# Decayed attention in a fused attention and two-MLP kernel: units of 64 steps of four batches on 64x64 tiles, and loops written out

## The reference

```python
def _attn_ref(r, k, v, w, u):            # (4, 8, 768, 48): batch, heads, steps, width
    for t in range(S):
        cur = einsum('bhd,bhe->bhde', u[None] * kt, vt)
        y[:, :, t] = einsum('bhd,bhde->bhe', rt, state + cur)
        state = wt[:, :, :, None] * state + einsum('bhd,bhe->bhde', kt, vt)
```

## Time and profile before

| | us |
|---|---|
| median of 3 runs | 892.63 (889.56 to 893.0) |
| span of the profiled execution | 889.9 |
| TensorE busy | 804.8 (90%), granted clock 0.973 |
| DVE, ACT, POOL busy | 527.3, 427.7, 181.4 |
| ACT's copies into `r_diag` | 116.6 (168 of them) |

### The profile page before, as it was taken

The page is one execution under the profiler, slowest core; times in us unless marked ns, Lnnn a source line. Parts: engine busy times, 40 slices in busy tenths (PEclk is TensorE's granted clock), DMA queues, the critical chain, the costliest instruction groups (busy, mean ns, idle before and its releaser), DMA issues.

```text
span 889.9 us, 23575 instructions
## 1 busy us (share of the span) xinstructions
PE 804.8 (90%) x9648; PEld 667.1 (75%) x9648; DVE 527.3 (59%) x906; ACT 427.7 (48%) x716; POOL 181.4 (20%) x189
## 2 busy tenths in 40 slices
PE   2365958999999999999999999899999999999998
PEld 2254848779779779779778778678878778887786
DVE  5657384783883883683783683584584674453333
ACT  4536354673573573473473473363463573342332
POOL 5223222221221221221221221132132131000000
PEclk9978887999999999999999999899999999999999
DMA  5140345147535434334434434344434432333653
GB/s 179 36 124 3 91 162 120 49 145 180 189 127 170 165 123 127 128 126 127 152 112 130 140 111 125 109 144 136 131 108 133 138 140 90 123 127 107 235 190 106
DMA packets 33971, 114.75 MB, mean 129 GB/s; under 512 B 5840, under 2 KB 14544, under 8 KB 33872
## 3 DMA queue, kind: packets, MB, share of 16 engines
q1 hardware_dynamic: 33872, 113.27, 40.7%
HBM read 91.23 MB, written 17.30 MB: 122 GB/s over the span
## 4 chain that ended last, share of the span: by engine, by line
PE 73%; DVE 12%; issue 6%; ACT 4%; POOL 1%; SPq 1%; DMA 1%; DVEq 0%; ACTq 0%; POOLq 0%
PE hid L492 20%; PE acc L505 17%; PE flex L476 12%; PE flex L445 10%; PE flex L375 3%; PE flex L413 3%; PE flex L416 3%; PE flex L459 2%; DVE r_t L618 2%; DVE att L600 2%; DVE solu L659 2%; PE flex L427 1%; ACT att L815 1%; DVE ln_lo L687 1%; DVE w_up L627 1%
## 5 line engine op out<-in xcount | busy, mean ns | idle before, releaser
L492 PE MATMUL hid<-y_hi,w 128*128 128x512 f32 x576 | 198.8, 399 | 3.2 <-DVE y_lo L694 3.2
L505 PE MATMUL acc<-g_hi,w 128*128 128x512 f32 x576 | 197.2, 396 | 1.4 <-DVE g_lo L703 0.9
L815 ACT ACTIVATE r_diag<-r_t 64x512 f32<-64x512 f32 (+1 forms) x168 | 116.6, 694 | 105.8 <-DVE r_t L618 89.7
L699 DVE TENSOR_TENSOR act<-act 128x512 f32<-128x512 f32 x96 | 73.6, 766 | 125.3 <-ACT g_hi L815 125.3
L1010 POOL TENSOR_TENSOR k_t<-k_t,w_up 128x512 f32<-128x512 f32 x72 | 87.4, 1213 | 220.5 <-PE flex L375 160.6
L492 PEld LDWEIGHTS hid<-y_hi,w 128*128 128x128 f32 x576 | 109.0, 189 | 27.2 <-issue 3.6
L505 PEld LDWEIGHTS acc<-g_hi,w 128*128 128x128 f32 x576 | 108.1, 188 | 26.6 <-issue 2.8
L815 ACT ACTIVATE act<-hid 128x512 f32<-128x512 f32 x96 | 57.3, 597 | 135.1 <-PE hid L492 134.9
L492 PE MATMUL hid<-y_lo,w 128*128 128x512 f32 x288 | 113.3, 393 | 0.0
L505 PE MATMUL acc<-g_lo,w 128*128 128x512 f32 x288 | 112.6, 391 | 0.0
L476 PE MATMUL flex<-ln_hi,out_hi 128*128 128x256 f32 x288 | 82.8, 288 | 0.0
(11 more groups left out here) (98 smaller groups left out, 1348.5 us busy)
## 6 DMA issues: line engine op xcount, KB each, us to landing
w<-split_w SPq DMA_DIRECT2D x80, 768.0 KB, 4.4
split_w<-w SPq DMA_DIRECT2D x16, 768.0 KB, 4.1
r_t<-in_rT SPq DMA_DIRECT2D x24, 192.0 KB, 4.9
k_t<-in_kT SPq DMA_DIRECT2D x24, 192.0 KB, 4.7
w_t<-in_wT SPq DMA_DIRECT2D x24, 192.0 KB, 5.6
v_n<-in_vN SPq DMA_DIRECT2D x12, 384.0 KB, 3.3
out<-o_stage SPq DMA_DIRECT2D x5, 768.0 KB, 4.1
x_pack<-x_t SPq DMA_DIRECT2D x72, 48.0 KB, 2.4
```

The source lines that it names most:

```text
L492: last = mm(hid[:, :], w2[:, j % RING, w, k * P:(k + 1) * P], y[:, k, :], start=n == 0, stop=n == len(terms) - 1)
L505: last = mm(acc[:, d], w2[:, j % RING, w, rows], gx[:, j % 2], start=j == 0 and n == 0, stop=j == J2 - 1 and n == 2, skip_group_check=True)
L699: e.tensor_tensor(act[:, j % 2], act[:, j % 2], act[:, j % 2], ALU.mult).then_inc(g_ready, 1)
L815: return nc.scalar.activation(out_, in_, func, **more)
```

## The change

A unit becomes 64 steps of all four batches: `T` = 64, `NU` = 12 units, `Q` = 16 blocks of 64 columns, six levels. All tiles keep their number of columns, the state loses its axis of pairs, and each unit now decays and updates all of it. `r_diag`, `att_bk`, `right_halves`, `take_level5`, `take_level6` and `place_blocks` go. The matmuls of the bonus and the levels read `r_t` and `k_t` themselves, one head each, on tiles of 64 rows and 64 columns; the head chooses the PSUM bank, the parity of `q` the column half. DVE masks each level (512 elements a partition, before 256; the bonus 1024, before 512) straight into `att`. `carry(l)` now stands behind `pair_scores(l)` and waits for the matmuls of its own level. One of the two output copies goes to ACT; `k_natural` waits for the last level's scores, `output` for both halves of k, `state_step` for both output copies. The first MLP's and the second MLP's matmuls stay as they are. The loops over blocks 1 to 3 are written out on every engine.

```diff
-T = 128
-LEVELS = 7
+T = 64
+LEVELS = 6
-LEVEL_AT = {1: 0, 3: 1, 4: 2, 6: 3, 7: 4, 8: 5, 9: 6}
+LEVEL_AT = {1: 0, 3: 1, 4: 2, 6: 3, 7: 4, 8: 5}
+        def scores(q, i):
+            return flex[HALF * (q % 2):HALF * (q % 2 + 1), i, q // 2 * T:(q // 2 + 1) * T]
...
             def bonus(u):
                 pe.wait_ge(uk_ready, u + 1)
-                pe.wait_ge(rdiag_ready, u * 14 + 2)
-                wait(pe, x_ready, u * 2)
+                pe.wait_ge(r_in, (u + 1) * 32)
+                wait(pe, state_ready, u * 2)
                 for q in range(Q):
...
+                    steps = slice(q * T, (q + 1) * T)
                     for i in range(2):
                         rows = slice(HALF * i, HALF * (i + 1))
+                        last = mm(scores(q, i), uk[rows, steps], r_t[rows, steps], start=True, stop=True)
+                last.then_inc(bonus_mm, 1)
+            def level(u, l):
+                if l == 0:
+                    pe.wait_ge(bonus_taken, u + 1)
+                else:
+                    pe.wait_ge(r_ready, u * LEVELS + l)
+                    pe.wait_ge(k_ready, u * LEVELS + l)
+                    pe.wait_ge(level_taken, u * LEVELS + l)
+                for q in range(Q):
+                    steps = slice(q * T, (q + 1) * T)
+                    for i in range(2):
+                        rows = slice(HALF * i, HALF * (i + 1))
+                        out_ = scores(q, i)[:, 0:T // 2].rearrange("p (n m) -> p n m", m=1 << l)
+                        last = mm(out_, k_t[rows, steps], halves(r_t[rows, steps], l)[:, :, 1, :], start=True, stop=True)
+                last.then_inc(level_mm, 1)
...
+            def output(u):
+                pe.wait_ge(r_ready, u * LEVELS + LEVELS)
+                pe.wait_ge(vn_in, (u + 1) * 16)
+                pe.wait_ge(knat_ready, (u + 1) * 2)
+                for q in range(Q):
+                    x, b2 = q // 2, q % 2
+                    for i in range(2):
+                        mm(flex[HALF * i:HALF * (i + 1), b2, x * T:(x + 1) * T], state[:, q, i], r_t[:, q * T:(q + 1) * T],
+                           start=x == 0, stop=False, skip_group_check=True)
+                for q in range(Q):
+                    x, b2 = q // 2, q % 2
+                    rows = slice(HALF * b2, HALF * (b2 + 1))
+                    for i in range(2):
+                        last = mm(flex[HALF * i:HALF * i + D, b2, x * T:(x + 1) * T], v_n[rows, x % NBH, head_cols(x, i)],
+                                  att[rows, i, x], start=False, stop=x == NX - 1, skip_group_check=True)
...
             def pair_scores(u, l):
...
+                v.wait_ge(level_mm, u * LEVELS + l + 1)
+                keep = mask[:, off:off + pairs].bitcast(U32).unsqueeze(1).unsqueeze(3).broadcast_to([P, Q, pairs, 1 << l])
                 e.copy_predicated(dst, keep, src).then_inc(level_taken, 1)
...
             def carry(u, l):
...
-                v.wait_ge(rdiag_ready, u * 14 + 2 * l + 2)
...
+                v.wait_ge(level_mm, u * LEVELS + l + 1)
                 right = halves(r_t[:, :], l)[:, :, 1, :]
...
             def attention(u, g, i):
-                if i in CARRY_AT:
-                    carry(u, CARRY_AT[i])
...
+                if i == 0:
+                    bonus_scores(u)
+                elif i in LEVEL_AT:
+                    pair_scores(u, LEVEL_AT[i])
+                    carry(u, LEVEL_AT[i])
...
-            with pe.Fori(1, NC - 2) as m:
+            for m in range(1, NC - 2):
                 block_turns(m)
```

More of the change, by code:

```diff
@@ L92, in build @@
         out_hi, out_lo = sb("out_hi", [P, J1, DM], F32R), sb("out_lo", [P, J1, DM], F32R)
-        state = sb("state", [P, G, Q, 2, HALF])
+        state = sb("state", [P, Q, 2, HALF])
         u_rows = sb("u_rows", [P, NP])
@@ L221, in load_r @@
             def load_r(u):
-                wait(sp, y_mm, u * 2)
+                wait(sp, y_mm, u)
                 for i in range(2):
@@ L365, in level @@
-                bank = flex[:, l % 2]
-                for q in range(Q):
[L367 to L384, removed]
@@ L398, in k_natural @@
                     last.then_inc(knat_mm, 1)
-            def output(u, g):
+            def output(u):
                 pe.wait_ge(r_ready, u * LEVELS + LEVELS)
-                pe.wait_ge(blocks_placed, (u + 1) * NBK)
                 pe.wait_ge(vn_in, (u + 1) * 16)
[L405 to L418, removed]
+                pe.wait_ge(knat_ready, (u + 1) * 2)
[7 more added lines that the diff above has]
+                    rows = slice(HALF * b2, HALF * (b2 + 1))
+                    for i in range(2):
+                        last = mm(flex[HALF * i:HALF * i + D, b2, x * T:(x + 1) * T], v_n[rows, x % NBH, head_cols(x, i)],
+                                  att[rows, i, x], start=False, stop=x == NX - 1, skip_group_check=True)
+                last.then_inc(y_mm, 1)
@@ L420, in state_step @@
             def state_step(u):
-                pe.wait_ge(x_ready, u * 2 + 1)
+                pe.wait_ge(x_ready, u * 2 + 2)
                 for q in range(Q):
-                    p, b = q // NB, q % NB
+                    x, b2 = q // 2, q % 2
+                    rows = slice(HALF * b2, HALF * (b2 + 1))
                     for i in range(2):
-                        rows = slice(HALF * i, HALF * (i + 1))
-                        last = mm(flex[rows, 0, q * D:(q + 1) * D], k_nat[:, q, rows], v_n[:, b, (2 * p + i) * D:(2 * p + i + 1) * D],
-                                  start=True, stop=True)
+                        last = mm(flex[HALF * i:HALF * (i + 1), b2, x * D:(x + 1) * D], k_nat[rows, x, HALF * i:HALF * (i + 1)],
+                                  v_n[rows, x % NBH, head_cols(x, i)], start=True, stop=True)
@@ L519, in attention @@
                 elif i == 11:
-                    output(u, g)
+                    output(u)
                 elif i == 12:
@@ L630, in take_output, with add_state @@
                 wait(v, packed, u * 16 * len(REPACK))
-                for half in range(2):
-                    v.wait_ge(y_mm, u * 2 + half + 1)
-                    e.tensor_copy(x_t[:, half * 512:(half + 1) * 512], flex[:, half]).then_inc(x_ready, 1)
-            def add_state(u, g):
+                v.wait_ge(y_mm, u + 1)
+                e.tensor_copy(x_t[:, :, 1, :], flex[:, 1].rearrange("p (a n) -> p a n", a=NP)).then_inc(x_ready, 1)
+            def add_state(u):
                 v.wait_ge(state_decayed, u * 2 + 2)
@@ L801, in _ @@
             block_turns(0)
-            with v.Fori(1, NC - 2) as m:
+            for m in range(1, NC - 2):
                 block_turns(m)
@@ L859, in take_k, with take_output @@
                     a(k_nat[:, 4 * half:4 * half + 4].rearrange("p q n -> p (q n)"), flex[:, half], ACT.Copy).then_inc(knat_ready, 1)
+            def take_output(u):
+                wait(s, packed, u * 16 * len(REPACK))
+                s.wait_ge(y_mm, u + 1)
+                a(x_t[:, :, 0, :], flex[:, 0].rearrange("p (a n) -> p a n", a=NP), ACT.Copy).then_inc(x_ready, 1)
             def x_high(u):
@@ L979, in _ @@
             block_turns(0)
-            with s.Fori(1, NC - 2) as m:
+            for m in range(1, NC - 2):
                 block_turns(m)
@@ L1017, in decay_state @@
                     rows = slice(HALF * i, HALF * (i + 1))
-                    st = state[rows, g, :, i, 0:D]
+                    st = state[rows, :, i, 0:D]
                     e.tensor_tensor(st, st, w_level(LEVELS, rows).unsqueeze(2).broadcast_to([HALF, Q, D]), ALU.mult)\
@@ L1051, in _ @@
                             pattern=[[-1, P]], channel_multiplier=1).then_inc(init_p, 1)
-            for l in range(IN_BK):
-                pairs = T >> (l + 1)
-                cols = steps_mask[:, T - 2 * pairs:T - pairs]
+            for l in range(LEVELS):
+                pairs = P >> (l + 1)
+                cols = steps_mask[:, P - 2 * pairs:P - pairs]
                 e.affine_select(out=cols, in_=cols, compare_op=ALU.is_ge, fill=0.0, base=0,
@@ L1076, in _ @@
             block_turns(0)
-            with pool.Fori(1, NC - 2) as m:
+            for m in range(1, NC - 2):
                 block_turns(m)
             block_turns(NC - 2)
-_LAYOUT_PAIRS = (G, NB, NP, 2, NC, T, D)
+_LAYOUT_PAIRS = (NBH, 2, NP, 2, NU, T, D)
 def kernel(r, k, v, w, u, moe_w_in, moe_w_out, moe_g_ln, moe2_w_in, moe2_w_out):
```

214 lines of the change are left out of this document (67 added, 147 removed).

## The result

The changed kernel takes 898.43 us (median; 897.71 to 901.59) against 892.31 in the same runs: ratio 1.0073, interval 1.0052 to 1.0094. It is slower by 6 us, 0.7%, and the interval excludes a ratio of 1; I had forecast 868.5, and 848 to 896 as the range. The profiled execution's span went from 889.9 to 896.3 us.

A forecast was written before the change was run, and what follows sets the result against it. TensorE was taken to bound the kernel from 160 us on, latencies before that. Full turns -5, start -13 and loops -6 sum to -24 us: span 889.9 to about 866, median 868.5, range 848 to 896.

The forecast's parts named there:

- The price of a 64x64 tile: TensorE's level matmuls: 12.5 ns an instruction, between bounds of 11 and 32 ns; all matmuls 0.55 us less a unit.
- The steady stall: Each turn's 1.02 us TensorE wait for DVE's normalisation before the transposes: would shrink, by less than the level-6 copies' 1.37 us.
- The first 160 us: Turns 0 to 2, where latencies count: 13 us less, bounds -22 and -2.
- the small cycle of turn 0: One level's matmul, mask and carry in turn 0: 3.3 to 3.6 us, from 4.72, with the matmul at 1.1.
- adds nothing: Start: the next bonus no longer waits for r_diag copies, but x_low, ahead of bonus_scores on DVE, is late next; no gain.
- both terms: Two mis-sized terms of the start: the level groups' price, and bonus_scores standing behind x_low on DVE.
- The loops: TensorE stops of 1.97 and 2.30 us in the bonus and slow `hid` go when unrolled: -6 us, bounds -7 and +2.
- Rival 2: 64x64 tiles do not overlap by rows in score, output and update matmuls: 32 ns an instruction, 965 us; chance 0.12.
- the floor of 25 ns: Skill's rule that matmul starts are never below about 25 ns apart: 16.7 us a unit, about 927 us.
- point of return, 18 ns: Instruction price from which nine turns of some 450 TensorE instructions eat the 24 us gain and the kernel turns slower.
- Rival 1: DVE's mask and carry collide with POOL's product and stall TensorE: 2 us more a turn, 891 us; chance 0.13.
- the level-2 cover: Shortest cover for DVE's chain, level 1 to level 2: nine matmuls, 2.3 us; it fits with some 0.6 us to spare.

The follow-up runs named there:

- experiment 5: Changed kernel with the bonus masked early in turns 1 and 2, plus the last level's mask and carry moved behind the second normalise: 887.18 us, 0.9944 of before.
- experiment 3: Changed kernel with DVE masking the bonus of turns 1 and 2 before x_low and the weight piece: 887.85 us, 0.9947 of before.
- experiment 4: Changed kernel with the early bonus mask in turns 1 and 2 and half the weights in every level, other scores left out: 861.43 us, 0.9657 of before.
- e1: Kernel before with only its loops over blocks 1 to 3 written out: 882.75 us, 0.9878 of before.

## Why the prediction was wrong

The profiled span came out 30 us above the forecast one: 15 in the start (2.2 longer where 13 less were forecast) and 15 behind it (4.2 longer where 11 less were).

**The price of a 64x64 tile** (the step "I take 12.5 ns"). It is 16.7 ns. I chose by number of tiles, moving columns and instructions, and did not ask whether the weights set the price, though I had named wider weights in the upper bound. The unit's matmuls are 6 x 1.07 + 1.09 + 3.05 + 1.02 = 11.6 us, not 10.3: 0.7 more than before in place of 0.55 less. The levels alone are 1.6 us over; the output (3.05 against 3.35 worked out) was 0.3 cheaper than I had it, and the state update was right. In nine turns the matmuls are 11 to 12 us of my error, and the same price adds to the start.

**The steady stall.** I had it shrink, since the level-6 copies leave DVE. It grew to 1.13 us a turn, against 0.37 in the written-out kernel before; in turns 3 and 4 it is 2.02 against 0.85. The last level's mask and carry ahead of the normalisation explain 0.4 of that (experiment 5). The rest is open; the one-column product that takes 0.99 us for 0.16 is the likeliest place. Against the written-out kernel the matmuls (0.7), this wait (0.86 on average of eight turns) and the stops at the output (0.1) make 1.7 us a turn, which is what the turns differ by (13.7 us in eight).

**The first 160 us.** Of the 13 us nothing came. The step that failed is the one in which the small cycle of turn 0 carried a matmul of 1.1 us (it was 1.93: the earlier trace rows' 1.08 was already the slow form of the old group; the cycle came out at 4.0 us, above my 3.6), and the one in turn 1 in which bonus_scores behind x_low "adds nothing": I had seen that order, but set it against the gain of the r_diag wait alone, and counted 3 us for the turn. It cost 7.9 us of waiting, and experiment 3 brought that wait down to 1.95. The transposes of turn 0 did come earlier, at 38.62 us for 42.01, not at 34.6. By the starts of the bonus turn 0 gained 2.7 us (52.19 for 54.93), turn 1 lost 4.6 and turn 2 lost 0.3, where I had counted gains of 7.4, 3 and 2.5. With both terms taken away the sum of the start was as forecast, its parts were not (experiment 4).

**The loops.** 9 us in place of 6 (11.1 in the eight turns, less a start 2.5 longer): the stops as predicted, and a shorter stall in all the looped turns, which I did not foresee.

**Rival 2 and the floor of 25 ns.** The page TensorE: Matmul & The Clock Gate of the Trainium skill ("Wait — 56ns, not 53.3ns?") would have made a level's group 1.6 us. Neither the 64x64 tiles (1.07) nor the 64x32 tiles (0.68) show it; with several tiles in turn the trace disagrees with it. My rival 2, row halves that do not overlap, fell too. The sign of the result was its sign, by another mechanism: its own point of return, 18 ns, rested on a start gain that did not come. **Rival 1** did not happen: no level in the full turns waited for the carry, the level-2 cover of about 2.3 us held. The collisions that it named are there, though: between 290 and 700 us a level's mask takes 0.92 us on average where I had 0.74, and a carry of r 0.91 where I had 0.68.

## What to carry to other kernels

When small fp32 matmuls are re-tiled, count the columns of weights per instruction as well as the tiles and the moving columns: here 64 instructions with 32 moving columns cost 0.7 us with 32 columns of weights and 1.07 with 64, and 64 moving columns made the cheap form cost 1.03. When a step is put in front of a dependent matmul on an in-order engine, list what stands ahead of it on that engine in the thinly filled turns too, since the order that is harmless under full cover costs the whole wait there. Take a change of several parts in pieces: the writing out alone gained 9 us, and the rest cost 16. And look at what DVE and POOL do at the same time, down to the smallest products.

## What the runs showed of the hardware that was not expected

- Sixty-four instructions on 64x64 tiles take 1.05, 1.07 or 1.09 us at 16, 32 or 64 moving columns. With 32 columns of weights they take 0.68 (64x32) or 0.71 us (128x32) at 32 moving columns, and 1.03 (128x32) at 64.
- A DVE product of one column takes 0.99 us, for 0.16, beside POOL's product for k_t, and ends with it (both at 398.7 us in the changed kernel); one of 16 columns takes 1.07 for 0.18.
- Loops written out shortened even turns without a stop, by 0.7 us (turns 5, 6 and 10).
- The start spread by 2.5 us between two kernels with the same code in it: the bonus of turn 3 at 157.70 us before and at 160.21 in e1, one profiled execution of each. Differences in the start of that size prove nothing.
